# List places for the last six token tiles in pairs, with two steps of the routing stage in another order

## The chip, the cores and the metric

The kernel runs on one core of a Trainium2 chip. The metric is the device time in microseconds (us) of one execution; the figure given for a kernel is the median of its runs.

## The reference

Three layers follow one another over N = 2304 tokens (4 batches of 576) of width 512:

```
k_p, v_p = means of k and v over groups of 8 keys           # 72 pooled keys a head
attn     = softmax(q @ k_p.T / 8) @ v_p                      # 8 heads of 64 -> x [2304, 512]
noisy    = x @ w_gate + log1p(exp(x @ w_noise)) * noise      # 8 experts
top2     = the two largest of noisy; weights = softmax over the two
x2       = sum over top2 of weight * relu(x @ w1[e]) @ w2[e] # only the chosen experts, F = 1024
out      = sum over 4 experts of p[e] * relu(x2 @ w1b[e]) @ w2b[e]
```

The first expert layer is sparse: each token goes to two of eight experts. All is float32; large products are made of three passes over high and low parts.

## The kernel before

Tokens are handled as 18 tiles of 128. The program has three stages, one behind the other on TensorE.

**Attention and routing (to about 128 us).** A hand-written loop over `s` runs from 0 to 19. In turn `s`, TensorE makes the scores of tile `s + 1`, turns the exponentials of tile `s`, makes the values of tile `s - 1` (`values`) and turns and projects tile `s - 2` to logits (`x_turn_a`, `logits`). VectorE subtracts maxima (`max_subtract(s + 1)`) and scales the output rows (`post(s - 1)`); ScalarE makes exponentials and copies (`x_copy`, `logit_copy` of tile `s - 2`).

Routing is done for groups of tiles, listed in `GROUPS`. For a group `(first, end)`:

- turn `end + 1`: `softplus` on ScalarE (L1152, L1154);
- turn `end + 2`: `select` on VectorE (L1519 to L1538): noisy logits, the two best experts, one-hot masks, running totals;
- turn `end + 3`: `ranks` on TensorE (L812 to L816) counts how many tokens ahead go to the same expert, `places` on VectorE (L1546 to L1553) makes the row of each token in its experts' lists, `second_exp` on ScalarE (L1159) and `pair_weights` on VectorE (L1559 to L1561) make the two weights;
- as soon as `places` has signalled, GpSimd's queue scatters the tiles of the group into `x_sorted` in HBM, two indirect DMAs a tile (`scatter`, L505), 36 in all, strictly in order of groups. It also waits for `x_ps` (how many tiles' values are done).

The last group is never handled inside the loop: its softplus, choice and places stand behind it, as do the places of any group whose turn `end + 3` is beyond turn 19. Each engine executes its program in the order written; there is no scheduler.

Beside routing, the loop prepares the weights of expert 0, in four quarters `r`: ScalarE makes the high part in one cast (`high_first(r)`, L1163, turns in `HIGH_AT`), VectorE the low part in two halves (`low_half(r, half)`, L1600, turns in `LOW_AT`). The second half of a low part signals `raw_used`; for quarter 2 this lets SyncE's queue load the first quarter of expert 1 into the same buffer (L334, 1 MB).

Behind the loop VectorE reads the counts (`cnt`, L1638 on), makes a table of tiles, the low parts of quarter 3, and the order of tokens (to L1702). ScalarE's queue waits until all 36 scatters have landed (L1206) and loads the first rows of the lists (L1207); TensorE turns them (L865), ScalarE makes the high part (L1214), VectorE the low part (`x_lo`, L1607), and TensorE begins the first expert layer.

**First expert layer (about 128 to 645 us).** A tile of 128 list rows is 24 matmuls up (L884), turns (L893, L865) and 24 matmuls down (L910). GpSimd splits the weights of experts 1 to 7 (L644, L647).

**Second expert layer (to the end).** Products of blocks of rows with units of weights (L944, L1043); VectorE adds the outputs (L1871).

The functions that the change touches, and what calls them, are these:

Of the kernel before, what the change touches and what calls it, by code (L numbers as in the profile page):

```python
# [32 lines left out]
XS = 10  # L33
Q_FIRST = 2 * P
K_HALF, V_HALF = 2 * SEQ, CHUNKS * POOL * HD // 2
GROUPS = ((0, 4), (4, 8), (8, 12), (12, 15), (15, 17), (17, 18))

TILES_B = 2 * N // P + EXPERTS - 1
SURE_TILES = 2 * N // P
# [43 lines left out]
def build(nc, q, k, v, w_gates, noise, w1, w2, probs, w1b, w2b, out):  # L83
# [5 lines left out]
    with ExitStack() as ctx:  # L89
# [185 lines left out]
        N_POOL_CONST = 15  # L275
        K_AT, V_AT = {2: 1, 5: 2, 9: 3}, {4: 1, 8: 2, 12: 3}
        V_BLOCKS_AT = {0: 0, 4: 1, 9: 2, 13: 3}
        HIGH_AT = {11: 0, 14: 1, 17: 2, 19: 3}
        LOW_AT = {13: ((0, 0), (0, 1)), 15: ((1, 0),), 16: ((1, 1),), 18: ((2, 0),), 19: ((2, 1),)}

        def real(eng, code):

# [166 lines left out]
        def _(pool):  # L449
# [38 lines left out]
            def kv_add(b, what):  # L488
                i = 2 * b + what
                pool.wait_ge(kv_in[i % 4], 16 * (i // 4 + 1))  # L490
                if what:
                    pool.dma_start(kv[0:QR, i % 4, :], v[b][:, V_HALF:2 * V_HALF], accum_op=ALU.add
                                   ).then_inc(kv_added[i % 4], 16)
                else:
                    pool.dma_start(kv[:, i % 4, 0:K_HALF], k[b][:, K_HALF:2 * K_HALF], accum_op=ALU.add
                                   ).then_inc(kv_added[i % 4], 16)

            def scatter(g):
                pool.wait_ge(pos_ok, g + 1)
                first, end = GROUPS[g]  # L500
                for t in range(first, end):

                    pool.wait_ge(x_ps, min(end + 3 + t - first, NT - 2))
                    for kk in range(2):
                        pool.indirect_dma_start(  # L505
                            x_sorted[:, :], bass.IndirectOffsetOnAxis(ap=pos_i[:, t, kk:kk + 1], axis=0),
                            x_sb[:, t % XS, :], None).then_inc(xs_out[t % XS], 16)

            for b in range(1, BATCH):
                kv_add(b, 0)  # L510
                kv_add(b, 1)
            for g in range(len(GROUPS)):
                scatter(g)
# [142 lines left out]
            pool.wait_ge(order_ok, 1)  # L656
            pool.wait_ge(wts_ok, len(GROUPS))
            pool.wait_ge(p_ok, 2)
# [92 lines left out]
        def _(pe):  # L751
# [45 lines left out]
            def logits(s):  # L797
                if s == 0:
                    pe.wait_ge(wg_in, 16)
                pe.wait_ge(aT_done, s + 1)  # L800
                for c in range(KD):
                    mm = pe.matmul(bank[0][:, 0:2 * EXPERTS], aT[:, c, :], wg[:, c, :], start=(c == 0), stop=(c == KD - 1))  # L802
                mm.then_inc(lg_ps, 1)

            def ranks(g):
                first, end = GROUPS[g]
                size = end - first
                pe.wait_ge(mask_ok, g + 1)
                if g:
                    pe.wait_ge(pos_ok, g)  # L810
                dst = rank_cols[:, 0:EXPERTS * size]
                pe.matmul(dst, upper[:, :], mask_b[:, first:end, :], start=True, stop=False, skip_group_check=True)  # L812
                for j in range(1, size):
                    pe.matmul(rank_cols[:, EXPERTS * j:EXPERTS * size], ones_b[:, :],
                              mask_b[:, first:end - j, :], start=False, stop=False, skip_group_check=True)
                pe.matmul(dst, ones_b[:, :],  # L816
                          total_b[:, g % 2:g % 2 + 1, :].to_broadcast([P, size, EXPERTS]),
                          start=False, stop=True, skip_group_check=True).then_inc(rank_ps, 1)

            scores(0)  # L820
            for s in range(NT + 2):
# [8 lines left out]
                if s >= 2:  # L830
                    logits(s - 2)
                for g, (first, end) in enumerate(GROUPS[:-1]):
                    if s == end + 3:
                        ranks(g)
            for g, (first, end) in enumerate(GROUPS[:-1]):
                if end + 3 >= NT + 2:
# [276 lines left out]
        def _(act):  # L1113
# [35 lines left out]
            def softplus(g):  # L1149
                first, end = GROUPS[g]  # L1150
                act.wait_ge(lg_ok, end)
                act.activation(nscale[:, first:end, :], lg[:, first:end, EXPERTS:], ACT.Exp).then_inc(sp_e, 1)  # L1152
                act.wait_ge(sp_e, g + 1)
                act.activation(nscale[:, first:end, :], nscale[:, first:end, :], ACT.Ln, bias=1.0).then_inc(sp_ok, 1)  # L1154

            def second_exp(g):
                first, end = GROUPS[g]
                act.wait_ge(rdiff, g + 1)
                act.activation(dexp[:, first:end], dif[:, first:end], ACT.Exp).then_inc(rexp, 1)  # L1159

            def high_first(r):
                act.wait_ge(raw_in[r % 2], 16 * (r // 2) + 16)
                act.copy(wall[:, 0, r // 2, 0, 2048 * (r % 2):2048 * (r % 2) + 2048], raw[:, r % 2, :]  # L1163
                         ).then_inc(split_no, 1)
# [3 lines left out]
            for s in range(NT + 2):  # L1168
# [10 lines left out]
                for g, (first, end) in enumerate(GROUPS[:-1]):  # L1179
                    if s == end + 1:  # L1180
                        softplus(g)
                    if s == end + 3:
                        second_exp(g)
                if s in HIGH_AT:
                    high_first(HIGH_AT[s])
            for g, (first, end) in enumerate(GROUPS[:-1]):
                if end + 3 >= NT + 2:
                    second_exp(g)
            softplus(len(GROUPS) - 1)
            second_exp(len(GROUPS) - 1)  # L1190

            codes = {}
# [236 lines left out]
        def _(dve):  # L1429
            done = [0]  # L1430

            def then(ins):

                done[0] += 1
                ins.then_inc(dstep, 1)
                dve.wait_ge(dstep, done[0])
# [104 lines left out]
            def places(g):  # L1541
                first, end = GROUPS[g]
                n = end - first
                span = slice(first, end)
                dve.wait_ge(rank_ps, g + 1)
                then(dve.tensor_tensor(  # L1546
                    place[:, 0:n, :], base8[:, :].rearrange("p (s e) -> p s e", s=1).to_broadcast([P, n, EXPERTS]),
                    rank_cols[:, 0:EXPERTS * n].rearrange("p (s e) -> p s e", s=n), ALU.add))
                then(dve.tensor_tensor(place2[:, 0:n, :, :], oh[:, span, :, :],
                                       place[:, 0:n, :].rearrange("p s (k e) -> p s k e", k=1).to_broadcast(  # L1550
                                           [P, n, 2, EXPERTS]), ALU.mult))
                then(dve.tensor_reduce(pos_f[:, 0:n, :], place2[:, 0:n, :, :], AX.X, ALU.add))
                dve.tensor_copy(pos_i[:, span, :], pos_f[:, 0:n, :]).then_inc(pos_ok, 1)  # L1553

            def pair_weights(g):
                first, end = GROUPS[g]
                span = slice(first, end)
                dve.wait_ge(rexp, g + 1)
                then(dve.tensor_scalar(dsum[:, span], dexp[:, span], 1.0, 1e-9, ALU.add, ALU.add))  # L1559
                then(dve.reciprocal(wts[:, span, 0], dsum[:, span]))  # L1560
                dve.tensor_tensor(wts[:, span, 1], dexp[:, span], wts[:, span, 0], ALU.mult).then_inc(wts_ok, 1)  # L1561
# [31 lines left out]
            def low_half(r, half):  # L1593

                at = slice(1024 * half, 1024 * half + 1024)
                hi = wall[:, 0, r // 2, 0, 2048 * (r % 2):2048 * (r % 2) + 2048]
                lo = wall[:, 0, r // 2, 1, 2048 * (r % 2):2048 * (r % 2) + 2048]
                if half == 0:
                    dve.wait_ge(split_no, r + 1)
                d = dve.tensor_tensor(lo[:, at], raw[:, r % 2, at], hi[:, at].bitcast(F32), ALU.subtract)  # L1600
                if half:
                    d.then_inc(raw_used[r % 2], 1)
# [10 lines left out]
            for s in range(NT + 2):  # L1613
# [8 lines left out]
                for g, (first, end) in enumerate(GROUPS[:-1]):  # L1622
                    if s == end + 2:
                        select(g)
                    if s == end + 3:
                        places(g)
                        pair_weights(g)
                for r, half in LOW_AT.get(s, ()):
                    low_half(r, half)
# [2 lines left out]
                places(g)  # L1632
            select(len(GROUPS) - 1)
            places(len(GROUPS) - 1)


            dve.wait_ge(cnt_ps, 1)
# [305 lines left out]
```

## Time and profile before

| | |
|---|---|
| median of three runs | 1407.44 us (1404.55 to 1409.35) |
| the profiled execution: its own time | 1407.4 us |
| the profiled execution: span, first to last instruction | 1405.7 us |
| mean granted TensorE clock | 0.988 |
| TensorE matmuls busy | 1346.4 us (96%) |
| VectorE, ScalarE, GpSimd busy | 700.8, 393.7, 693.6 us |

All times inside the kernel are from the span's start. PE is TensorE, PEld its weight loads, DVE VectorE, ACT ScalarE, POOL GpSimd, SP SyncE; a q behind a name is that engine's sequencer or DMA queue. In square brackets behind a timeline row stands how long the engine was idle before it and what ended that. Ends of matmuls are modelled, so a matmul row that overlaps the next is normal.

### The profile page before, as it was taken

How to read it: one execution, taken by the hardware profiler on the slowest of the kernel's cores; microseconds unless marked ns; L12 is line 12 of the kernel's file. 1: busy time of each engine (PE TensorE's matmuls, PEld its weight loads, DVE VectorE, ACT ScalarE, POOL GpSimd, SP SyncE). 2: the span in 40 equal slices, each digit the busy share in tenths (PEclk: the TensorE clock that was granted, in tenths of full speed). 3: DMA queues.
4: the chain of work that ended last, by engine and by line, in shares of the span. 5: the costliest groups of instructions: out<-in, count | busy, mean ns of one | idle time of the engine just before them, and what ended most of it. 6: DMA issues, size and time to landing. Idle time of an engine off the chain costs nothing.

```text
span 1405.7 us, 21984 instructions
## 1 busy us (share of the span) xinstructions
PE 1346.4 (96%) x6985; PEld 1184.0 (84%) x6986; DVE 700.8 (50%) x1292; ACT 393.7 (28%) x736; POOL 693.6 (49%) x464
## 2 busy tenths in 40 slices
PE   5994999999999999998999999999999999999997
PEld 5993878888888888887789899898999899889986
DVE  5886321122222212315876775865555555655564
ACT  2561212122222221413344343422222222322210
POOL 1343688356382737696866786433332222233202
PEclk9996999999999999999999999999999999999999
DMA  9945275243232425213322322201110100001002
GB/s 265 293 181 195 77 250 165 67 134 104 98 134 75 164 72 190 85 55 104 99 82 75 106 90 90 90 30 31 40 51 30 30 30 30 30 30 39 6 0 90
DMA packets 63605, 133.72 MB, mean 95 GB/s; under 512 B 5496, under 2 KB 23048, under 8 KB 63448
## 3 DMA queue, kind: packets, MB, share of 16 engines
q1 hardware_dynamic: 43320, 84.69, 18.5%
q0 software_dynamic: 8272, 26.49, 5.8%
q10 hardware_dynamic: 11952, 21.76, 4.7%
q8 instruction: 33, 0.54, 0.2%
q14 instruction: 28, 0.23, 0.0%
HBM read 108.22 MB, written 30.74 MB: 99 GB/s over the span
## 4 chain that ended last, share of the span: by engine, by line
PE 89%; DVE 3%; issue 2%; DMA 1%; POOL 1%; ACT 1%; another core or an unknown queue 1%; SPq 0%; ACTq 0%; DVEq 0%; POOLq 0%
PE banks L1043 27%; PE banks L944 24%; PE banks L884 15%; PE banks L910 15%; PE banks L893 2%; POOL x_sorted L505 1%; PE banks L865 1%; PE banks L784 1%; PE banks L762 1%; DMA kv_half<-in_v 1%; DVE hD L1828 1%; PE banks L772 1%; PE banks L802 1%; PE banks L794 0%
## 5 line engine op out<-in xcount | busy, mean ns | idle before, releaser
L1043 PE MATMUL banks<-unit_w,hD 128*128 128x512 f32 x1728 | 404.7, 391 | 3.2 <-DVE acc L1871 2.6
L1043 PEld LDWEIGHTS banks<-unit_w,hD 128*128 128x128 f32 x1728 | 322.3, 188 | 72.8 <-DVE acc L1871 7.0
L944 PE MATMUL banks<-x_ops,unit_w_hi 128*128 128x384 f32 x1344 | 342.6, 335 | 7.8 <-issue 4.2
L944 PEld LDWEIGHTS banks<-x_ops,unit_w_hi 128*128 128x128 f32 x1344 | 243.2, 188 | 13.6 <-issue 7.4
L1871 DVE SCALAR_TENSOR_TENSOR acc<-banks,sorted_record,acc 128x512 f32<-128x512 f32 x270 | 200.3, 748 | 104.7 <-PE banks L1043 100.8
L884 PE MATMUL banks<-expert_w,xT 128*128 (+1 forms) x960 | 232.3, 398 | 1.5 <-DVE xT L1607 1.5
L538 POOL TENSOR_TENSOR unit_w_lo<-raw_weights,unit_w_hi 128x512 fp32r<-128x512 f32 (+1 forms) x60 | 62.8, 1068 | 337.9 <-ACT unit_w_hi L1372 337.9
L910 PE MATMUL banks<-expert_w,hT 128*128 (+1 forms) x960 | 224.9, 390 | 0.6 <-issue 0.6
L944 PE MATMUL banks<-x_ops,unit_w_lo 128*128 128x384 f32 x672 | 225.1, 335 | 0.0
L884 PEld LDWEIGHTS banks<-expert_w,xT 128*128 128x128 f32 x960 | 179.7, 191 | 38.7 <-issue 2.0
L910 PEld LDWEIGHTS banks<-expert_w,hT 128*128 128x128 f32 x960 | 180.0, 188 | 38.3 <-issue 1.1
L1738 DVE COPY y_rows<-banks 128x512 f32<-128x512 f32 x40 | 27.6, 691 | 331.9 <-PE banks L910 323.5
L644 POOL TENSOR_TENSOR expert_w<-raw_weights,zeros 128x2048 f32 x28 | 100.8, 3601 | 162.6 <-PE banks L910 138.2
L647 POOL TENSOR_TENSOR expert_w<-raw_weights,expert_w 128x2048 f32 x28 | 128.9, 4602 | 5.2 <-POOL expert_w L644 5.2
L944 PEld LDWEIGHTS banks<-x_ops,unit_w_lo 128*128 128x128 f32 x672 | 126.1, 188 | 0.0
L1828 DVE SCALAR_TENSOR_TENSOR hD<-block_sums,hD 128x384 fp32r<-128x384 f32 x144 | 95.9, 694 | 28.6 <-ACT hD L1356 28.4
L1232 ACT CAST hT<-banks 128x512 fp32r<-128x512 f32 x80 | 43.0, 590 | 189.3 <-PE banks L893 184.0
L1223 ACT ACTIVATE h_rows<-banks 128x512 f32<-128x512 f32 x80 | 43.5, 595 | 184.7 <-PE banks L884 168.0
L542 POOL TENSOR_TENSOR unit_w<-raw_weights,unit_w 128x1024 fp32r<-128x1024 f32 x31 | 75.7, 2441 | 27.6 <-ACT unit_w L1378 27.6
L1354 ACT COPY block_sums<-banks 128x384 f32<-128x384 f32 x48 | 23.0, 480 | 205.1 <-PE banks L944 200.0
L1727 DVE TENSOR_TENSOR hT<-banks,hT 128x512 fp32r<-128x512 f32 x80 | 51.5, 686 | 50.2 <-ACT hT L1232 48.9
L538 POOL TENSOR_TENSOR unit_w_lo<-weight_sums,unit_w_hi 128x1024 fp32r<-128x1024 f32 x30 | 74.0, 2466 | 0.0
(232 smaller groups left out, 1273.0 us busy)
## 6 DMA issues: line engine op xcount, KB each, us to landing
raw_weights<-in_w SPq DMA_DIRECT2D x32, 1024.0 KB
raw_weights<-in_w1b SPq DMA_DIRECT2D x32, 512.0 KB
raw_weights<-in_w2b SPq DMA_DIRECT2D x32, 512.0 KB, 3.4
x_rows<-x_sorted ACTq DMA_DIRECT2D x43, 256.0 KB
y_sorted<-y_rows ACTq DMA_DIRECT2D x40, 256.0 KB
qT<-in_q SPq DMA_DIRECT2D x3, 1152.0 KB, 19.6
kv_half<-in_k SPq DMA_DIRECT2D x5, 576.0 KB, 11.6
kv_half<-in_v SPq DMA_DIRECT2D x5, 576.0 KB, 11.3
```

The lines of the kernel that those rows point to most:

```text
L538: ins = pool.tensor_tensor(lo, src, hi.bitcast(F32), ALU.subtract)
L542: pool.tensor_tensor(w2o[par][:, 1, :], raw[:, par, 1024:2048], w2o[par][:, 0, :].bitcast(F32), ALU.subtract).then_inc(w2_ok, 1)
L644: pool.tensor_tensor(hi, src, zeros[:, 0:1].to_broadcast([P, 2048]), ALU.add).then_inc(split_no, 1)
L647: pool.tensor_tensor(lo, src, hi.bitcast(F32), ALU.subtract).then_inc(raw_used[r % 2], 1)
L884: mm = pe.matmul(bank[n][:, :], xT[:, u % 2, st, c, :], wall[:, bass.ds(slot, 1), 0, mv, FF * c + 512 * n:FF * c + 512 * n + 512], start=( ...
L910: mm = pe.matmul(bank[5 + u % 2][:, :], hT[:, u % 2, st, c, :], wall[:, bass.ds(slot, 1), 1, mv, D * c:D * c + D], start=(t == 0), stop=(t ...
L944: mm = pe.matmul(dst[:, 0:HALF], (w1h, w1l)[st][par][:, b, c, :], x2o[blk][:, a, mv, c, :], start=(first and t == 0), stop=(t == 5), skip_ ...
L1043: mm = pe.matmul(bank[5 + t % 3][:, :], hD[:, buf, st, c, P * t:P * t + P], w2o[par][:, mv, D * c:D * c + D], start=(n == 0), stop=(n == 3 ...
L1223: r = act.activation(h_sb[:, 512 * n:512 * n + 512], bank[n][:, :], ACT.Relu)
L1727: d = dve.tensor_tensor(hT[:, u % 2, 1, 4 * n:4 * n + 4, :], bank[2 + n][:, :].rearrange("p (c r) -> p c r", c=4), hT[:, u % 2, 0, 4 * n:4 ...
L1828: dve.scalar_tensor_tensor(out=hD[:, buf, 1, m, at:at + HALF], in0=src, scalar=0.0, in1=hD[:, buf, 0, m, at:at + HALF].bitcast(F32), op0=A ...
L1871: dve.scalar_tensor_tensor(out=to, in0=bank[5 + t % 3][:, :], scalar=p, in1=to, op0=ALU.mult, op1=ALU.add).then_inc(acc_ok, 1)
```

## The change

The tiles 12 to 17, until now in groups of three, two and one tiles, are in three groups of two. Two steps are placed elsewhere: the high part of quarter 3 on ScalarE is made behind the last softplus instead of in turn 19, and the second half of the low part of quarter 2 on VectorE is made behind the last group's choice and places instead of in turn 19.

```diff
--- before.py
+++ after.py
@@ -33,7 +33,7 @@
 XS = 10
 Q_FIRST = 2 * P
 K_HALF, V_HALF = 2 * SEQ, CHUNKS * POOL * HD // 2
-GROUPS = ((0, 4), (4, 8), (8, 12), (12, 15), (15, 17), (17, 18))
+GROUPS = ((0, 4), (4, 8), (8, 12), (12, 14), (14, 16), (16, 18))
 
 TILES_B = 2 * N // P + EXPERTS - 1
 SURE_TILES = 2 * N // P
@@ -275,8 +275,8 @@
         N_POOL_CONST = 15
         K_AT, V_AT = {2: 1, 5: 2, 9: 3}, {4: 1, 8: 2, 12: 3}
         V_BLOCKS_AT = {0: 0, 4: 1, 9: 2, 13: 3}
-        HIGH_AT = {11: 0, 14: 1, 17: 2, 19: 3}
-        LOW_AT = {13: ((0, 0), (0, 1)), 15: ((1, 0),), 16: ((1, 1),), 18: ((2, 0),), 19: ((2, 1),)}
+        HIGH_AT = {11: 0, 14: 1, 17: 2}
+        LOW_AT = {13: ((0, 0), (0, 1)), 15: ((1, 0),), 16: ((1, 1),), 18: ((2, 0),)}
 
         def real(eng, code):
 
@@ -1187,6 +1187,7 @@
                 if end + 3 >= NT + 2:
                     second_exp(g)
             softplus(len(GROUPS) - 1)
+            high_first(3)
             second_exp(len(GROUPS) - 1)
 
             codes = {}
@@ -1632,6 +1633,7 @@
                 places(g)
             select(len(GROUPS) - 1)
             places(len(GROUPS) - 1)
+            low_half(2, 1)
 
 
             dve.wait_ge(cnt_ps, 1)
```

By the rules of the loop, the softplus, choice and places of tiles 12 and 13 fall in turns 15, 16 and 17 (before, with tile 14, in 16, 17 and 18). Those of tiles 14 and 15 fall in turns 17, 18 and 19 (before, tile 15 with tile 16 had softplus in turn 18, choice in 19 and places behind the loop). Tiles 16 and 17 are handled behind the loop (before, tile 17 alone).

## Rows read from the trace of the kernel before

**Rows 1.** The page: groups of TensorE's matmuls, busy and idle before.

```profile
...
L1043 PE MATMUL banks<-unit_w,hD 128*128 128x512 f32 x1728 | 404.7, 391 | 3.2 <-DVE acc L1871 2.6
...
L884 PE MATMUL banks<-expert_w,xT 128*128 (+1 forms) x960 | 232.3, 398 | 1.5 <-DVE xT L1607 1.5
```

**Rows 2.** Chain that ended last, 104 to 140 us: start, length, what.

```profile
...
105.61 2.19 issue
...
122.61 2.72 DMA x_sorted<-x_sb,pos_int
...
125.72 2.75 DMA x_rows<-x_sorted
...
131.12 7.72 PE banks L884 x24
...
156.74 5.47 PE banks L884 x24
```

**Rows 3.** Timeline of GpSimd: scatters of token rows.

```profile
...
108.02 0.96 POOL L505 DMA_INDIRECT x_sorted<-x_sb,pos_int  x1 [2.42 <-DVE pos_int L1553]
109.29 0.97 POOL L505 DMA_INDIRECT x_sorted<-x_sb,pos_int  x1 [0.30 <-issue]
```

**Rows 4.** Timeline of VectorE, 98 to 116 us.

```profile
...
98.42 1.21 DVE L1600 TENSOR_TENSOR expert_w<-raw_weights,expert_w 128x1024 fp32r<-128x1024 f32 x1
100.93 0.17 DVE L1473 TENSOR_SCALAR row_sums<-banks 128x8 f32<-128x8 f32 x1 [1.29 <-PE banks L784]
...
105.85 0.17 DVE L1473 TENSOR_SCALAR row_sums<-banks 128x8 f32<-128x8 f32 x1 [1.79 <-PE banks L784]
...
107.58 0.17 DVE L1553 CAST pos_int<-pos_float 128x6 int32<-128x6 f32 x1
...
108.14 1.22 DVE L1600 TENSOR_TENSOR expert_w<-raw_weights,expert_w 128x1024 fp32r<-128x1024 f32 x1
109.28 0.22 DVE L1519 TENSOR_TENSOR noisy_logits<-noisy_logits,noise_sb 128x16 f32<-128x16 f32 x1
...
111.06 1.22 DVE L1600 TENSOR_TENSOR expert_w<-raw_weights,expert_w 128x1024 fp32r<-128x1024 f32 x1
112.20 0.16 DVE L1546 TENSOR_TENSOR place<-list_base,banks 128x16 f32<-128x16 f32 x1
...
112.84 0.25 DVE L1553 CAST pos_int<-pos_float 128x4 int32<-128x4 f32 x1
...
114.51 0.16 DVE L1546 TENSOR_TENSOR place<-list_base,banks 128x8 f32<-128x8 f32 x1
...
115.66 0.17 DVE L1638 TENSOR_SCALAR cnt<-banks 128x8 f32<-128x8 f32 x1 [0.35 <-PE banks L841]
```

**Rows 5.** Timeline of VectorE, ahead of the first tile.

```profile
...
130.28 0.69 DVE L1607 TENSOR_TENSOR xT<-banks,xT 128x512 fp32r<-128x512 f32 x1 [2.63 <-ACT xT L1214]
```

**Rows 6.** Timeline of ScalarE.

```profile
...
110.36 1.90 ACT L1163 CAST expert_w<-raw_weights 128x2048 fp32r<-128x2048 f32 x1
```

**Rows 7.** Timeline of TensorE.

```profile
...
107.04 0.66 PE L794 MATMUL banks<-ident,x_sb 128*128 128x128 f32 x4 [1.17 <-DVE x_sb L1477]
108.37 1.89 PE L802 MATMUL banks<-gate_w,x_sbT 128*128 128x16 f32 x8 [0.68 <-ACT x_sbT L1143]
...
114.26 0.19 PE L812 MATMUL banks<-mask_b,upper 128*128 128x8 bf16 x1 [3.13 <-DVE mask_b L1533]
```

**Rows 8.** Timeline of SyncE's queue.

```profile
...
112.31 0.37 SPq L334 DMA_DIRECT2D raw_weights<-in_w  x1
```

**Rows 9.** Stretches: length, busy of each engine, clock, DMA share, GB/s.

```profile
...
108.00:110.00 2.00, 1.63 (x8) 1.64 (x8) 1.87 (x7) 0.31 (x1) 1.67 (x2) 0.53 0.31 119
118.00:120.00 2.00, 0.00 (x0) 0.00 (x0) 1.86 (x8) 0.00 (x0) 1.39 (x3) 0.50 1.03 416
122.00:124.00 2.00, 0.00 (x0) 0.00 (x0) 1.93 (x4) 0.00 (x0) 1.27 (x2) 0.50 0.45 170
130.00:135.00 5.00, 3.88 (x9) 3.14 (x10) 4.24 (x23) 0.25 (x1) 0.00 (x0) 0.50 0.63 250
```

## The prediction, made before the changed kernel was run

> **What bounds the kernel now.** I read the page's groups first. TensorE is busy for 96% of the span, and the matmuls of both expert layers had almost nothing to wait for: L884 was idle for 1.5 us in all, L1043 for 3.2 [rows 1]. So from the first tile of the first expert layer on the time is TensorE's own work, and a change in routing can act in one way only: by moving the start of that work. The chain of work that ended last tells what sets the start. From some 30 us ahead of the first expert tile it leaves TensorE and runs along GpSimd's scatters, then the landing of the last of them (2.72 us), the load of the first list rows (2.75 us), and then the matmuls of L884 [rows 2]. The reader is to see in it one break: 2.19 us of "issue" from 105.61 us, ahead of a scatter at 108.02 us whose row says that GpSimd had waited 2.42 us for `pos_int`, the places of group 3 [rows 2, 3]. Elsewhere scatter follows scatter at about 1.275 us (0.97 busy and 0.30 between, as at 109.29). So the scatters are a chain with one hole in it, and each group's places must be there when the chain comes to it.
>
> **The change part by part.**
>
> *Group 3 becomes tiles 12 and 13, a turn earlier.* Its choice stands behind the `post` that ended about 98.4 us. A choice for two tiles lasts from 109.28 to 111.06, 1.78 us [rows 4], so it is done at 100.2; its ranks follow in turn 17, and its places come behind the `post` of 100.93, so at about 103. The chain of scatters needs them at 105.61. The hole goes: the next scatter starts at 105.61 + 0.30 = 105.91 instead of 108.02, **2.11 us earlier**.
>
> *Group 4 becomes tiles 14 and 15, with places in turn 19.* After four scatters GpSimd is ready for it at 105.91 + 4 x 1.275 = 111.01. When are its places made? The `post` of tile 17 starts at 105.85 and ends near 106.9, as before. Then come its choice (1.78 us, to 108.7) and the half low part that was at 108.14 (1.14 us to the next row, to 109.8) [rows 4]. Its ranks are now queued on TensorE behind the logits of tile 17, which start at 108.37 and last 1.89 us [rows 7], at a granted clock of 0.50 to 0.56 in that stretch, the lower of its two levels (1.2 GHz) [rows 9]; so they start near 110.2. From a rank matmul (114.26) to the places that read it (114.51) is 0.25 us; places for two tiles take 112.20 to 113.09, 0.89 us [rows 4, 7]; from places to scatter is 0.27 us (107.75 to 108.02) [rows 3, 4]. That gives 110.2 + 0.25 + 0.89 = 111.35 for the places and 111.6 for the scatter. The hole of 2.11 us is replaced by one of **about 0.6 us** in front of group 4. Bounds: 0 (the ranks come 0.6 us sooner) to 1.6 us (they come a us later). Net of both, 1.5 us.
>
> *The last group is two tiles, with ScalarE's cast behind its softplus.* The cast of quarter 3 (110.36, 1.90 us) stood between the last logit copy and the last softplus, which could start no sooner than 112.26 [rows 6]. Now the softplus is done by about 111.1. VectorE comes to the last choice at 111.35 (places of group 4) + 0.4 (weights, as from 107.75 to 108.14) = 111.75; choice to 113.5, then 0.25 for the ranks and 0.9 for the places, to about 114.7 [rows 4, 7]. Before, they ended near 115.3, ahead of the counts at 115.66. GpSimd asks for them at 111.6 + 4 x 1.275 = 116.7: no wait. The cast itself moves from 110.36 to 111.1 and ends at 113.0; nobody reads quarter 3 until VectorE's low parts, which stand behind the counts (115.66): free, with 2.6 us of cover at least, and were it late, VectorE's next low part would be.
>
> *The half low part behind the last places.* It keeps its 1.14 us on VectorE, and ends at about 115.8 instead of 112.2. The counts behind it start at 115.8 instead of 115.66 [rows 4]: VectorE is 0.2 us later for everything up to the token order. That is covered: VectorE was idle 2.63 us before the first `x_lo` [rows 5]. The cover caps the gain, though: with `x_lo` wanted more than 2.6 - 0.2 = 2.4 us earlier, VectorE is the last to be ready.
>
> *The load that this releases.* SyncE's load of 1 MB waits for that half. It was issued at 112.31, beside the scatters [rows 8]; now at about 115.8, 3.5 us later. The DMA engines were full from 118 to 120 us (share 1.03, 416 GB/s) and at 0.45 from 122 to 124 [rows 9], that is, they had just come free when the last scatter (122.61) was issued. Moved by 3.5 us, the full stretch reaches to about 124, over the landing of the last scatter and up to the load of the first rows. The chain shows 2.72 and 2.75 us for these two under a light load; no row shows them under a full one. Bounds: 0, if they share freely, and 1.05 MB at 416 GB/s = 2.5 us, if all of the load goes ahead of them. I take **0.6 us**, nearer to the low end, because the load has some 5 us (115.8 to 121) to land in before the last scatter is issued. The Trainium skill ("Trainium Kernel Development and Optimization", Key Constraints) speaks against the change here: DMAs of the SP, ACT and POOL queues all run on the same 16 engines and interleave. The rows agree in so far as share and rate rise together while both are under way; by a fair interleaving alone the term would be some tenths of a us for each of the two.
>
> *Small things in the loop.* The choice of group 3 now stands ahead of the half low part of 98.42 us: that ends at 98.4 + 1.78 + 1.14 = 101.3 instead of 99.6, and the next `post`, at 100.93, is 0.4 us late [rows 4]. TensorE's next step waits for that `post`, but the following `post` (105.85) had waited 1.79 us for other things, which covers it. On ScalarE a softplus and a small exponential, three activations, go ahead of a cast in turn 17, and the copy of `x_sbT` behind that cast comes later by them; at the 0.2 us or so that I give each, an estimate, 0.6 us, and TensorE had 1.17 us to spare ahead of its next tile (107.04) [rows 7]. Cost 0, upper bound 0.6 us. A low part on VectorE did not slow the scatter beside it (0.96 us at 108.02, with a half of 1.22 us from 108.14 on), so where the moved half lies beside scatters costs nothing [rows 3, 4].
>
> **The sum.** 2.11 - 0.6 - 0.6 = 0.9 us gained. Against the profiled execution's own 1407.4 us that is 1406.5; that execution stands on the median (1407.44), so the forecast for the median is also **1406.5 us**. The three runs before spread over 4.8 us, and 0.3% (4.2 us) is about what a measurement can tell from no change.
>
> **Rivals.**
>
> *More of the gain arrives* (chance 0.2). The ranks of group 4 come in time and the later load costs nothing: 2.11 us, against the cap of 2.4. Time 1405.3. For it: a place that is only 0.6 us late is within my error. Against: TensorE's half clock in that stretch.
>
> *The later load takes the gain and more* (0.2), the case on the other side. If all of the 1.05 MB goes ahead of the last scatter or of the first rows, 2.5 us against 1.5 gained: 1408.4. It decides as soon as the two landings together (2.72 and 2.75) grow by more than 1.5 us.
>
> *The groups wait as before* (0.1). Ranks of group 3 or 4 sit behind a late choice on TensorE, and the hole only moves from group 3 to group 4: at 1.6 to 2.1 us in front of group 4, time 1407.4. That is the case in which the change does not do what it says.
>
> *The start of the expert layer meets TensorE's clock otherwise* (0.1). The first up-projection took 7.72 us where later ones took 5.47, with the clock granted at 0.50, the lower level, from 130 to 135 us [rows 2, 9]. TensorE's idle time ahead of it hardly changes, so I expect it to be slow again; where the clock rises can differ by up to those 2.2 us in either direction: 1404.3 to 1408.7.
>
> My forecast of 1406.5 has 0.4, its own range being 1405.6 to 1407.2. More than 4.2 us either way needs several of these in one direction and the spread between runs: faster by over 0.3% 0.07, within 0.3% 0.89, slower 0.04. The range takes in both bounds (2.5 us or so each way) and the spread of a median of a few runs: 1404.0 to 1409.0.
>
> **What would show it.** The first scatter of tile 12 at about 105.9 with no wait for places, the fifth after it (tile 14) at about 111.6 behind a wait of 0.5 to 0.7 us; the last scatter issued near 121.1 instead of 122.61 (the 1.5 us of net gain); SyncE's load issued near 116; landings slightly over 2.72 and 2.75; VectorE's idle before `x_lo` shrunk to about 1.5 us; the first L884 near 130.2; everything behind it shifted alike. It is wrong if the first L884 starts earlier than 128.8 or later than 131.1, or if something behind it (a wait for weights of expert 1, whose first quarter now comes later) opens on TensorE.

## The result and the profile after

The changed kernel took **1411.88 us** (median of 8 runs, 1411.33 to 1414.56), the kernel before **1408.01 us** beside it (8 runs, 1404.55 to 1409.72). The ratio is 1.0036, interval 1.0026 to 1.0047: slower by 0.36%, outside my range. The two profiled executions agree: spans 1409.6 and 1405.7 us. The page's groups behave as [rows 1]: the matmuls of both expert layers hardly wait, so the loss must sit ahead of the first expert tile.

```profile
L1043 PE MATMUL banks<-unit_w,hD 128*128 128x512 f32 x1728 | 404.9, 391 | 3.9 <-DVE acc L1873 3.3
...
L884 PE MATMUL banks<-expert_w,xT 128*128 (+1 forms) x960 | 231.1, 396 | 1.5 <-DVE xT L1608 1.5
```

The chain of work that ended last, of the changed kernel, from 103 us on (start, duration, what), against [rows 2]:

```profile
103.33 3.20 issue
...
106.77 0.97 POOL x_sorted L505
...
111.58 4.50 issue
...
116.30 0.97 POOL x_sorted L505
...
125.42 4.43 DMA x_sorted<-x_sb,pos_int
...
130.25 2.78 DMA x_rows<-x_sorted
...
135.68 7.68 PE banks L884 x24
...
147.49 5.64 PE banks L884 x24
```

The chain of scatters had one hole of 2.19 us; it now has two, of 3.20 and 4.50 us, ahead of groups 3 and 4. The last scatter is issued at 125.42 instead of 122.61 and lands in 4.43 instead of 2.72 us. The first matmuls of the expert layer start 4.56 us later (135.68 against 131.12): 2.81 us from the last issue, 1.71 from its landing. And this though everything up to 97 us ran 1.45 us earlier in this execution. About 1.4 us come back in the first two tiles, where the granted clock stayed at 1.00 for the second one (143 to 146 us; 0.55 before in the same stretch); the spans differ by 3.9 us.

What starts it is in the timelines of TensorE, VectorE and ScalarE in turn 17 (the bracket is the idle time before a row and what ended it):

```profile
97.94 1.52 PE L784 MATMUL banks<-v_blocks,expT 96*128 96x132 f32 x12
99.57 1.07 PE L802 MATMUL banks<-gate_w,x_sbT 128*128 128x16 f32 x8
100.48 0.17 PE L812 MATMUL banks<-mask_b,upper 128*128 128x16 bf16 x1
```

```profile
98.71 1.22 DVE L1601 TENSOR_TENSOR expert_w<-raw_weights,expert_w 128x1024 fp32r<-128x1024 f32 x1
104.63 0.17 DVE L1474 TENSOR_SCALAR row_sums<-banks 128x8 f32<-128x8 f32 x1 [4.70 <-remote]
104.72 0.17 ACT L1147 COPY logits<-banks 128x16 f32<-128x16 f32 x1 [5.21 <-remote]
```

TensorE was given tile 16's values at 97.94 us (modelled end 99.46), tile 15's logits at 99.57 and the ranks of group 3 at 100.48. VectorE waits for the first, ScalarE for the second, and both go on only at 104.63 and 104.72: the trace has the three signals (semaphore updates) at 104.61, 104.70 and 104.75 us, 4 to 5 us late and all at once. The releaser is given as "remote" because no row ends near that time. Whether the matmuls themselves or only their signals were late the trace can't tell, since their ends are modelled; "late signal" below means either. I call this **the stand**. TensorE in turn waits 5.12 us for VectorE's scaled rows, and then its clock falls. First the changed kernel, then one stretch of the kernel before:

```profile
core 0: us, PE busy (x) PEld busy (x) DVE busy (x) ACT busy (x) POOL busy (x), PEclk, DMA share, GB/s
100.00:102.00 2.00, 0.70 (x9) 0.60 (x8) 0.00 (x0) 0.00 (x0) 1.70 (x2) 1.00 0.67 161
102.00:104.00 2.00, 0.00 (x0) 0.00 (x0) 0.00 (x0) 0.00 (x0) 1.03 (x2) 0.56 0.85 238
104.00:106.00 2.00, 0.18 (x1) 0.19 (x2) 1.26 (x5) 1.24 (x5) 0.00 (x0) 0.50 1.02 387
106.00:108.00 2.00, 2.00 (x10) 2.00 (x10) 0.83 (x6) 1.66 (x2) 0.97 (x1) 0.50 0.58 231
```

```profile
106.00:108.00 2.00, 0.66 (x4) 0.42 (x4) 1.79 (x9) 0.91 (x5) 0.00 (x0) 1.00 0.95 379
```

In the kernel before the granted clock was 1.00 up to 108 us and 0.53 in the next 2 us [rows 9]. So the values and logits of tile 17 and the ranks of group 4 ran at 1.2 GHz (granted 0.50; tile 17's values took 2.85 us instead of 1.52), and VectorE waited again (2.65 us ahead of tile 17's division, 1.60 us for the ranks of group 4, whose places were made at 115.20). That is the second hole.

The landing of the last scatter is the other loss. In this stretch of the DMA view of the changed kernel only SyncE's load (q1) has packets; the scatters (q0) have none, though GpSimd issued one at 121.41 us and one at 122.78:

```profile
DMA packets 137, 0.56 MB, mean 281 GB/s; under 512 B 0, under 2 KB 0, under 8 KB 137
## 3 DMA queue, kind: packets, MB, share of 16 engines
q1 hardware_dynamic: 137, 0.56, 84.9%
```

(122 to 124 us.) From 121.5 to 125.0 us all 221 packets are q1's, and those of the scatters issued meanwhile follow from 125 us on. Before, the stretch from 122 to 124 us held 115 packets, all of q0. The Trainium skill ("Trainium Kernel Development and Optimization", Key Constraints) says that DMAs of these queues interleave on the 16 engines; over these 3.5 us the trace shows no sign of it.

### The profile page after: what moved, and what is told of

Read it like the earlier page. It is cut to its first block, busy times and chain, and to the rows that moved or that the text cites. A ratio compares the mean times of both kernels' runs of the same rounds, so it can differ in the third digit from the quotient of the medians.

```text
span 1409.6 us, 21984 instructions
## 1 busy us (share of the span) xinstructions
PE 1346.5 (96%) x6985; PEld 1183.6 (84%) x6986; DVE 703.5 (50%) x1292; ACT 393.6 (28%) x736; POOL 693.6 (49%) x464
## 4 chain that ended last, share of the span: by engine, by line
PE 88%; DVE 4%; issue 2%; DMA 1%; POOL 1%; ACT 1%; another core or an unknown queue 1%; SPq 0%; ACTq 0%; DVEq 0%; POOLq 0%
PE banks L1043 26%; PE banks L944 24%; PE banks L884 15%; PE banks L910 15%; PE banks L893 2%; POOL x_sorted L505 1%; PE banks L865 1%; PE banks L784 1%; DVE hD L1830 1%; PE banks L762 1%; DMA kv_half<-in_v 1%; PE banks L772 1%; PE banks L802 1%; DVE acc L1873 1%
## 5 line engine op out<-in xcount | busy, mean ns | idle before, releaser
L884 PE MATMUL banks<-expert_w,xT 128*128 (+1 forms) x960 | 231.1, 396 | 1.5 <-DVE xT L1608 1.5
L884 PEld LDWEIGHTS banks<-expert_w,xT 128*128 128x128 f32 x960 | 178.7, 189 | 38.8 <-issue 2.4
```

Source lines behind the costliest of these rows:

```text
L884: mm = pe.matmul(bank[n][:, :], xT[:, u % 2, st, c, :], wall[:, bass.ds(slot, 1), 0, mv, FF * c + 512 * n:FF * c + 512 * n + 512], start=( ...
```

## The experiments

I write a kernel's ratio to the kernel before with its 95% interval. The kernels of one set ran on one chip beside the kernel before, and the sets ran on different chips, which turned out to matter. Each kernel has one profile.

**First set: which part.** (a) The new groups alone; (b) the two moves alone; (c) the change with the load released ahead of the stand cut from 1 MB to 32 KB, so that quarter 3 of expert 0's weights is wrong; (d) the change with the load of expert 1's first quarter held until the first rows are back.

```
(a) GROUPS = (..., (12, 14), (14, 16), (16, 18)); HIGH_AT, LOW_AT as before
(b) GROUPS as before; high_first(3) and low_half(2, 1) behind the loop
(c) - load_raw(3, 0, 3, 1)
    + sp.wait_ge(raw_used[1], 1)
    + sp.dma_start(raw[:, 1, 0:64], w2[0, 512:512 + P, 0:64]).then_inc(raw_in[1], 16)
(d) - if r == 1:                      # expert 1's quarters
    + if r == 0:
          sp.wait_ge(xg_in[0], 16)
```

> The groups of two tiles alone; casts and low parts of the weights stay where they were before. Theory F (the first loss is code that VectorE and ScalarE fetch while SyncE's 1 MB load of quarter 3 fills the DMA engines; the second is the last scatter's landing behind the load that the moved half low part releases): VectorE's program is here in the same order up to turn 18 as in the changed kernel, so it stands still from about 100 to 104.6 us as there; the last scatter lands in about 2.7 us, since the other load goes out early. Time about 1410, 0.15% slower than before. Rival W (the wait sits in the ranks and places of the new groups, not in code): the same stand comes too, but only with the order of the two moved steps; then no stand here, 1407 or less. Rival L (the later load is the whole loss): 1406.5 here.

> The two moved steps alone, with the groups of before. Theory F: no stand of VectorE near 100 us; pause near 104 us as before (1.8 us); the load now goes out near 116 us and the last scatter lands in about 4.4 us instead of 2.7: about 1409.5, 0.1% slower. Rival L: all of the loss is here, 1412. Rival W: 1408, no change.

> The changed kernel, but SyncE's third-quarter load (512 rows x 512 columns of w2 for quarter 3 of expert 0) brings only 128 x 64 elements, so that expert 0 computes with wrong weights there; this takes away the suspected cost. Theory F: VectorE's and ScalarE's stand of 4.7 and 5.2 us at 100 us goes (below 1 us), places of tiles 12 and 13 by 103 us, no wait of GpSimd ahead of tile 12, wait ahead of tile 14 below 1 us, first L884 at about 131 us instead of 135.7: about 1407. Rival S (the stand is a semaphore or a place in the program, whatever the DMA engines do): the stand stays at 4.7 us and the time at 1411 to 1412.

> The changed kernel, but SyncE holds the load of expert 1's first quarter until the first list rows are in, so that it is in nobody's way at the last scatters. Theory F: the stand at 100 us stays, the last scatter lands in 2.7 us instead of 4.43, first L884 at about 134: 1410. Rival L: 1406.5. If a light and a full DMA load land alike: 1412, no change against the changed kernel.

Measured, with the kernel before at 1408.15 us: (a) 1.0024 (1.0013 to 1.0036), (b) 1.0005 (0.9995 to 1.0016), (c) 1.0038 (1.0021 to 1.0054), (d) 1.0025 (1.0013 to 1.0036). The stand is in (a), (c) and (d), as these rows of VectorE show, one of each, and not in (b):

```profile
108.00 0.17 DVE L1473 TENSOR_SCALAR row_sums<-banks 128x8 f32<-128x8 f32 x1 [4.66 <-remote]
```

```profile
105.43 0.17 DVE L1475 TENSOR_SCALAR row_sums<-banks 128x8 f32<-128x8 f32 x1 [4.61 <-remote]
```

```profile
107.67 0.17 DVE L1474 TENSOR_SCALAR row_sums<-banks 128x8 f32<-128x8 f32 x1 [4.62 <-remote]
```

```profile
100.30 0.17 DVE L1474 TENSOR_SCALAR row_sums<-banks 128x8 f32<-128x8 f32 x1 [1.29 <-PE banks L784]
```

So the new groups bring the loss, the moves nothing that can be told. The load of 1 MB under way in the stand is not its cause: with 32 KB instead it is as long. That answers theory F, by which VectorE and ScalarE stood for program text fetched behind this load. The packets of the instruction queues in the DMA view (q8, q14) do not mark the stand either: the one of q8 came at 98.9 us in the changed kernel, ahead of it, but at 107.9 in (c), behind it. Holding the other load let the last scatter land in 3.39 us instead of 4.43, but its ratio stands inside the interval of (a). In (b) I had expected a landing of 4.4 us, and it took 2.73, with the load issued 8.3 us ahead of the last scatter.

**Second and third set: place in the program, or order of the work.** Either the ranks of group 3 behind the transposes of turn 18, or 16, 64 or 128 empty instructions ahead of TensorE's first scores, so that everything behind stands elsewhere in its program; then the changed kernel and the kernel before once more as controls, and the shift together with (d).

```
ranks_later   in turn 18, behind x_turn_a(16):  ranks(3)      # not at the end of turn 17
nops_N        for _ in range(N): pe.nop()
              scores(0)
shift_hold    nops_64 and (d)
```

> TensorE's products for the places of group 3 (three small bf16 products) move from the end of turn 17 to turn 18, behind the four transposes of tile 16; VectorE and the groups stay as in the changed kernel. Theory S (TensorE's stand of 4 to 5 us comes when the ranks stand as the last work of a turn ahead of its next wait): nothing is withheld there, VectorE's idle ahead of tile 16's division (4.70 us) falls to 1 us or less, the clock stays up longer, and the span falls by 2 to 3.5 us against the changed kernel, to 1406 to 1408. Theory P (the stand belongs to a place in TensorE's program, counted in instructions from its start): the stand stays, since no instruction ahead of that place is added or removed but six; VectorE's idle stays at 4 to 5 us, and the span at 1409 to 1411.

> The changed kernel with 64 empty instructions on TensorE's queue ahead of its first scores, where it waits for the first quarter of the inputs anyway; all else is the same. Theory P (the stand belongs to a place in TensorE's program): the stand comes about a turn earlier or goes elsewhere, so VectorE's idle of 4.70 us ahead of tile 16's division and ScalarE's of 5.21 us ahead of the logits of tile 15 are gone or under 1.5 us, or a like idle stands in another turn; the time changes by up to 3.5 us, most likely down to 1408. Theory S (the stand comes from the order of TensorE's work, ranks of group 3 in turn 17): both idles stay at 4 to 5 us, and the time stays within 1 us of 1411.9.

> The kernel before with 64 empty instructions on TensorE's queue ahead of its first scores. Theory P: the short burst of late signals at 105.8 us (late by 1.3 us) moves, and may grow to a stand of several us in some turn; the time may then rise to 1411. Theory S: nothing changes; no stand over 1.5 us anywhere ahead of the tile work, and the time stays within 1 us of 1408.

> The changed kernel with 128 empty instructions on TensorE's queue ahead of its first scores. Theory P: the stand is in another place than with none and with 64, or is gone. Theory S: VectorE's idle ahead of tile 16's division stays at 4 to 5 us in turn 17.

Measured, with the kernel before at 1404.07 us: ranks_later 1.0003 (0.9991 to 1.0015), nops_64 0.9998 (0.9987 to 1.0009), nops_64_before 1.0004 (0.9989 to 1.0019), nops_128 1403.13 us in a single run. No stand in any of the four. I first read this as theory P confirmed. It was not, as the controls of the next set showed:

> The changed kernel once more, as the control for the runs with empty instructions, which ran on another chip than the first ones. If the stand of TensorE belongs to the program and its place (theory P): ratio 1.002 to 1.005, VectorE's idle of 4 to 5 us ahead of tile 16's division is there. If it belongs to the chip or the hour (theory H): ratio within 0.001 of 1, no idle over 1.5 us there, and the kernels with empty instructions showed nothing.

> The kernel before, profiled on the same chip as the changed one. Theory P: the burst of late signals in turn 18 (1.3 us) is there as in the first profile, the last scatter within 0.5 us of 25.5 us after tile 16's first product. Theory H: it depends on the chip; no burst here.

> The changed kernel with 64 empty instructions on TensorE's queue ahead of the first scores, and SyncE's load of expert 1's first quarter held until the first rows of x are back, so that no weight load runs beside the last scatters' landing. Forecast by theory P: no stand, all 18 scatters close behind each other, the last landing in 2.2 us instead of 3.0; ratio to the kernel before 0.998 to 1.000. Theory L (the later load costs nothing when the scatters flow): as with the 64 alone, 0.9998, within 0.0005. By theory H the ratio is that of the changed kernel, within 0.001.

> The changed kernel with 16 empty instructions ahead of TensorE's first scores. Theory P with a narrow place: no stand in turn 17 (idles under 1.5 us). Theory P with a wide place: the stand is there, 3 to 5 us. Theory S (order of work alone): the stand is there.

Measured, with the kernel before at 1402.99 us: the changed kernel itself 1.0004 (0.9992 to 1.0016) and **without a stand**; shift_hold 1.0006 (0.9993 to 1.0018), with the last landing in 2.71 us where I had expected 2.2 and a ratio of 1.000 at most; in single runs before_again 1404.96 and nops_16 1403.53 us, neither with a late signal. These rows are the changed kernel's there, in turns 17 and 18:

```profile
99.31 0.16 DVE L1474 TENSOR_SCALAR row_sums<-banks 128x8 f32<-128x8 f32 x1
...
102.53 0.17 DVE L1474 TENSOR_SCALAR row_sums<-banks 128x8 f32<-128x8 f32 x1 [0.64 <-PE banks L784]
```

So there are chips on which TensorE's signals are never late ahead of the expert layer, and the same program shows no loss on them. Theory H holds, and the fixes of the second set had nothing to fix.

**Fourth set: the two fixes again.** It ran on a chip where the kernel before takes 1407.92 us.

> The changed kernel with 64 empty instructions ahead of TensorE's first scores, once more. What is to be seen depends on the chip, by the runs so far: where the kernel before takes 1403 us or so, no stand and ratio 1.000 within 0.001, whatever the theory. Where it takes 1408: theory P (a place in TensorE's program) says no idle of VectorE over 1.5 us ahead of tile 16's division, and a ratio of 0.9995 to 1.001; theory S (the order of the work) says the idle of 4 to 5 us is there and the ratio 1.002 to 1.004.

> The changed kernel with the ranks of group 3 behind the transposes of turn 18, once more. Where the kernel before takes 1403 us or so: no stand, ratio 1.000 within 0.001. Where it takes 1408: theory S says the long stand is gone (VectorE's idle ahead of tile 16's division under 1.5 us) and the ratio 0.9995 to 1.001; theory P says that the stand stays at 4 to 5 us, ratio 1.002 to 1.004.

Measured: shift_again 1.0028 (1.0015 to 1.0041), ranks_again 1.0040 (1.0022 to 1.0058), both with the stand:

```profile
108.08 0.17 DVE L1476 TENSOR_SCALAR row_sums<-banks 128x8 f32<-128x8 f32 x1 [4.75 <-remote]
```

```profile
106.25 0.17 DVE L1476 TENSOR_SCALAR row_sums<-banks 128x8 f32<-128x8 f32 x1 [4.79 <-remote]
```

Neither the place in TensorE's program (for this shift) nor the ranks' place matters. In ranks_again TensorE's program is the kernel before's up to turn 18. What is left of the change ahead of the stand is what VectorE and ScalarE do: softplus and choice of group 3 a turn earlier.

**Fifth and sixth set: group 3 a turn later.** turn_later keeps the pairs but gives group 3 the turns that it had before; low_ahead only swaps VectorE's half low part and the choice of group 3 in turn 16.

```
turn_later   if s == end + (g == 3) + 1: softplus(g)      # and so for select, ranks, places, second_exp
low_ahead    LOW_AT without 16; in turn 16 low_half(1, 1) ahead of select(3)
```

> The changed kernel with the new groups, but softplus, choice, ranks and places of group 3 (tiles 12 and 13) one turn later, where the kernel before has those of its group 3 (tiles 12 to 14). Theory E (the stand comes with the earlier choice, that is with what VectorE and ScalarE do in turns 16 and 17): where the kernel before takes 1408 us, VectorE's idle ahead of tile 16's division falls from 4.7 us to 1.3 us or less, and the ratio to 0.9995 to 1.001. Theory C (the stand depends on the chip and the hour, and the two profiles with the old groups missed it by luck): the idle of 4 to 5 us is there, ratio 1.002 to 1.004. Where the kernel before takes 1403 us: no stand, ratio 1.000 within 0.001, which tells neither.

> The changed kernel with VectorE's half low part of turn 16 ahead of the choice of group 3 instead of behind it. Theory E with the order as its cause: the stand is gone, ratio 0.9995 to 1.001 where the kernel before takes 1408 us. Theory E with the choice's time as its cause, and theory C: the stand of 4 to 5 us stays, ratio 1.002 to 1.004. Where the kernel before takes 1403 us: no stand, ratio 1.000 within 0.001.

The fifth set met a chip of the other kind (before 1402.63 us): turn_later 1.0015 (1.0005 to 1.0025), low_ahead 0.9993 (0.9984 to 1.0003), no stand in either. Why turn_later is 0.15% slower there, above the 1.001 that I had allowed, stays open. The sixth met one with late signals (before 1408.01 us):

> The new groups with all steps of group 3 one turn later, once more. Where the kernel before takes 1408 us: theory E (the earlier choice brings the stand) says VectorE's idle ahead of tile 16's division is 1.3 us or less and the ratio 1.000 to 1.002 (1.0015 where no kernel has the stand); theory C (chance) says an idle of 4 to 5 us and a ratio of 1.003 to 1.005. Where it takes 1403 us: no stand, ratio 1.0005 to 1.0025 as in the last call.

> The changed kernel with the half low part of turn 16 ahead of the choice of group 3, once more. Where the kernel before takes 1408 us: if the order of the two brings the stand, no idle over 1.5 us ahead of tile 16's division and a ratio of 0.9985 to 1.0005; otherwise the idle of 4 to 5 us and 1.002 to 1.004. Where it takes 1403 us: no stand, ratio 0.9985 to 1.0005.

Measured: turn_later 0.9997 (0.9984 to 1.0011), low_ahead 1.0026 (1.0014 to 1.0037). In turn_later VectorE and ScalarE wait in turns 17 and 18 no longer than in the kernel before; in low_ahead the stand has moved from turn 17 to ScalarE's logits of turn 18. The rows of the first, then of the second:

```profile
99.65 0.17 DVE L1474 TENSOR_SCALAR row_sums<-banks 128x8 f32<-128x8 f32 x1 [1.29 <-PE banks L784]
...
102.99 0.17 DVE L1474 TENSOR_SCALAR row_sums<-banks 128x8 f32<-128x8 f32 x1 [0.49 <-PE banks L784]
...
105.18 0.17 ACT L1147 COPY logits<-banks 128x16 f32<-128x16 f32 x1 [1.79 <-PE banks L802]
```

```profile
100.58 0.17 ACT L1147 COPY logits<-banks 128x16 f32<-128x16 f32 x1 [1.31 <-PE banks L802]
...
103.91 0.17 DVE L1474 TENSOR_SCALAR row_sums<-banks 128x8 f32<-128x8 f32 x1 [1.45 <-PE banks L784]
...
108.18 0.17 ACT L1147 COPY logits<-banks 128x16 f32<-128x16 f32 x1 [4.65 <-remote]
```

All profiles together:

| sets in which the kernel before takes | group 3 in turns 16 and 17 | group 3 a turn later (or old groups) |
|---|---|---|
| 1408 us (the result, sets 1, 4, 6) | 7 profiles, in all of them VectorE or ScalarE idle for 4.6 to 5.2 us behind a signal 3 to 5 us late; ratios 1.0024 to 1.0040 | 3 profiles, signals of turns 17 and 18 late by 0.6 to 1.4 us; ratios 0.9997 and 1.0005 |
| 1403 to 1404 us (sets 2, 3, 5) | 7 profiles, none late; ratios 0.9993 to 1.0006 | 3 profiles, none late; ratios 1.0004 and 1.0015 |

No version tried was faster than the kernel before by more than its interval, on either kind of chip.

## Why the prediction was wrong

**The step that failed** is "its ranks follow in turn 17, and its places come behind the `post` of 100.93, so at about 103". The hole of 2.11 us was to go. On the chip of the result TensorE's signal for that `post` came 5 us late. GpSimd had been ready at 103.33 and scattered at 106.77 us, and the clock that fell in the stand made group 4 late too: GpSimd was idle for 3.43 and 4.73 us, 3.13 and 4.43 above the usual 0.30, where I had 0 and 0.6. The cause is shown as far as this: on chips with late signals, the steps of group 3 a turn earlier make a lateness of 0.6 to 1.4 us one of 3.5 to 5 us (7 profiles against 3), and moving those steps back takes the loss away (0.9997, beside 1.0026 for low_ahead on the same chip, with intervals that do not meet). What inside TensorE holds the signals, and why VectorE's and ScalarE's earlier choice makes it longer, stays open; the load's size, the shift in the program and the ranks' place were tried and are not it.

**A sign was in the rows of before.** I wrote of tile 17's `post` that it "had waited 1.79 us for other things". Its values were given to TensorE at 102.97 and last 1.52 us, to 104.49; the `post` began at 105.85 [rows 4], 1.36 us after their end:

```profile
102.97 1.52 PE L784 MATMUL banks<-v_blocks,expT 96*128 96x132 f32 x12
```

On a chip without late signals the same wait is nil and the hole is 0.96 us, not 2.42:

```profile
103.29 0.17 DVE L1473 TENSOR_SCALAR row_sums<-banks 128x8 f32<-128x8 f32 x1
...
105.72 0.97 POOL L505 DMA_INDIRECT x_sorted<-x_sb,pos_int  x1 [0.96 <-DVE pos_int L1553]
```

So some 1.4 of the 2.11 us that I meant to gain were not the groups' doing at all. A wait that its releaser's own row does not explain was to be priced as a rival.

**The sum where there is no stand.** In the third set, on a chip without late signals, the hole goes as forecast, and group 4 does not wait: its ranks ran at a granted clock of 1.00 (105 to 107 us), and tile 17's logits took 1.06 us and not 1.89. Counted from TensorE's transposes of turn 17 (96.27 us in after_again, 97.38 in before_again), the last scatter is issued at 22.50 us against 22.94, has landed at 25.45 against 25.66, and the first L884 starts at 31.18 against 31.32: 0.44 us gained in the chain, 0.21 left after the landing, 0.14 at the matmuls. The chain of after_again:

```profile
105.66 1.70 POOL x_sorted L505
...
116.82 1.64 POOL x_sorted L505
...
118.77 2.96 DMA x_sorted<-x_sb,pos_int
```

Two terms were mis-sized. The hole of 0.96 us is 0.66 more than the usual 0.30. And scatters closer together are not all 1.275 us apart: single issues take 1.6 to 1.7 us. I had 2.11 - 0.6; it was 0.4. The medians say 1.0004.

**The later load**: the mechanism was right, and my 0.6 us was too small. SyncE's load was issued at 120.23 us, 5.19 us ahead of the last scatter (125.42). That is the distance of my forecast (115.8 to 121), so the stand does not excuse the term: the landing rose by 1.71 us (4.43 against 2.72), within my bounds of 0 to 2.5. The profiles agree. Where the load is issued 5.2 us ahead of the last scatter (five of them), that lands in 4.13 to 4.67 us; where it is 7.1 to 10.3 us ahead (thirteen), in 2.72 to 3.22. All five have the stand, but so has (a), where the load is 7.6 us ahead and the landing takes 3.22. Not all of the 1.71 us is the load's: with the load held back in (d) the landing still took 3.39. I had also misread a row of before: the DMA engines full from 118 to 120 us [rows 9] moved the scatters (252 of 254 packets are q0's), not the load, so there was no full stretch of the load's to be moved over the landing. With the first rows at 2.78 us the two landings grew by 1.74, just over the 1.5 at which the rival built on the load was to take the gain. Even so it was not what decided: the moves alone gave 1.0005, and with the load held back in (d) the loss stayed (1.0025).

**The small things**: ScalarE's cast, the half low part and the order in turn 16 cost nothing measurable by themselves. "TensorE's idle time ahead of it hardly changes, so I expect it to be slow again" held: the first up-projection took 7.68 us. That the clock would rise at another time was a rival of mine, with 0.1: the second tile took 5.64 us and not 6.55, which with its transposes hid 1.4 us of the loss.

**What would show it**: the bound that I gave for being wrong (first L884 later than 131.1 us) was passed, at 135.68. The chance for slower by over 0.3% was 0.04. It left no room for a new wait at a place without a priced row; the largest number in my list of bounds was 2.5 us.

## What to carry to other kernels

Before a hole is counted as gain, follow its releaser back row by row: time between the end of the releasing row and the start of the waiting one is not the schedule's, and it can grow when the schedule is pulled tighter. A stop of TensorE can cost twice, once by itself and once by the lower clock granted behind it (0.50 from 104 us on, here). And an experiment needs its control on the same chip: here two fixes looked proved by runs on a chip that had nothing to mend.

## What the runs showed of the hardware

- **Chips differ in late signals of TensorE.** With the result and in sets 1, 4 and 6 (before at 1408 us) each of ten profiles has signals late by 0.6 to 1.5 us near 60 us, most have them near 79 us, and all between 105 and 108 us; in sets 2, 3 and 5 (before at 1403 to 1404 us) none of ten profiles has any ahead of the expert layer. The new groups are not needed for a long lateness: in the kernel before's profile the signal of work that TensorE was given at 121.33 us came at 125.27, where nobody waited for it (3.9 us; 0.2 in before_again). What makes up the 5 us between the medians is not settled. In the kernel before ScalarE waits 10.02 us for the up-projection at 204.71 us, where the other kind shows 4.36 us, but TensorE itself was idle for only 1.32 us there (to 205.85).
- **The late signals come out at nearly the same time, however early they are held.** In nine of the ten profiles those for VectorE and ScalarE come 8.7 to 9.5 us after TensorE was given the last logits of turn 16 (95.69 us in the changed kernel, 97.14 in the kernel before); what differs is the first work held back, given at 97.94 us in the one and at 102.97 in the other. In low_ahead ScalarE's came 12.2 us after it.
- **Beside a 1 MB load on SyncE's queue GpSimd's scatters can be without a packet** for 3.5 us at a time: 121.5 to 125.0 us above, and likewise 101.5 to 104.5 us (340 packets, all q1, behind scatters issued at 101.08 and 102.36). In the second stretch VectorE executed nothing, so it was not VectorE's work that held the scatters up.
